# Attention with a top-32 mask, a PReLU MLP and a switch MoE on one core: ScalarE's exponentials of a pass's first group move from behind the third probability tile to behind the first

## The reference, cut to what matters

```
scores = q @ k.T / sqrt(64)                       # 4 batches x 8 heads, 576 x 576
kth    = the 32nd largest of each row
attn   = exp(scores - max) where scores >= kth, else 0
attn   = attn / (sum(attn) + 1e-9)
x      = attn @ v                                 # becomes 2304 x 512
h      = x @ w_in;  g = max(h,0) + alpha*min(h,0); x2 = g @ w_out     # 512 -> 2048 -> 512
out    = x2 (+ gate * expert_e(x2) for the rows whose skip score is positive, one of 8 experts)
```

## Time and profile before

| | |
|---|---|
| median of three runs | 1118.12 us |
| profiled execution, its own time | 1123.2 us |
| its span (first to last instruction) | 1121.4 us |
| mean granted TensorE clock | 0.934 of 2.4 GHz |
| busy: PE, DVE, ACT, POOL | 927.9, 903.8, 631.4, 427.4 us |
| shares of the span | 83%, 81%, 56%, 38% |
| idle of DVE before L1070 for the exponentials of L844 | 5.9 us in 9 waits |
| idle of PE before L560 for POOL's L1324 | 34.4 us in 19 waits |

### The profile page before, as it was taken

The page is one execution under the profiler, slowest core; times in us unless marked ns, Lnnn a source line. Parts: engine busy times, 40 slices in busy tenths (PEclk is TensorE's granted clock), DMA queues, the critical chain, the costliest instruction groups (busy, mean ns, idle before and its releaser), DMA issues.

```text
span 1121.4 us, 22533 instructions
## 1 busy us (share of the span) xinstructions
PE 927.9 (83%) x6271; PEld 616.9 (55%) x6272; DVE 903.8 (81%) x1984; ACT 631.4 (56%) x1324; POOL 427.4 (38%) x598
## 2 busy tenths in 40 slices
PE   5346588898899889888988898899888889498996
PEld 2223256675666657665766575667556567243342
DVE  4999989999999999999999999999999270611110
ACT  3786969647855785587459637954883281010100
POOL 0136738514830682267028513840582100201110
PEclk9956589999999999999999999999999799699999
DMA  7910110013002200310031004001100166626650
GB/s 205 365 37 22 32 34 22 23 41 87 0 21 70 57 0 21 96 32 21 1 97 30 21 8 119 1 21 53 44 2 1 55 226 213 221 90 225 199 165 18
DMA packets 98658, 84.05 MB, mean 75 GB/s; under 512 B 69116, under 2 KB 77308, under 8 KB 98048
## 3 DMA queue, kind: packets, MB, share of 16 engines
q1 hardware_dynamic: 94544, 78.56, 23.0%
q0 software_dynamic: 1488, 3.15, 0.8%
q10 hardware_dynamic: 2528, 1.18, 0.4%
HBM read 72.64 MB, written 11.53 MB: 75 GB/s over the span
## 4 chain that ended last, share of the span: by engine, by line
PE 62%; POOL 12%; issue 11%; ACT 8%; DVE 4%; DMA 2%; POOLq 1%; ACTq 0%; DVEq 0%
PE acc L604 16%; PE acc L571 8%; PE sc L542 7%; PE pt_full L560 6%; PE acc L590 5%; POOL pos_part L358 5%; PE sc L712 3%; PE pt_full L772 3%; POOL arena L360 3%; POOL arena L1324 2%; PE pt_full L780 2%; PE sc L721 2%; PE acc L613 2%; ACT arena L844 1%; PE acc L619 1%
## 5 line engine op out<-in xcount | busy, mean ns | idle before, releaser
L1050 DVE MAX8 best<-arena 128x8 f32<-128x576 f32 x576 | 403.5, 742 | 9.8 <-ACT arena L835 6.6
L1063 DVE MATCH_REPLACE8 arena<-best,arena 128x576 f32<-128x576 f32 x432 | 315.8, 738 | 0.0
L1324 POOL TENSOR_SCALAR arena<-arena,row_inv 128x576 f32<-128x576 f32 x144 | 106.5, 757 | 351.3 <-DVE row_inv L1082 351.3
L590 PE MATMUL acc<-arena 128*128 (+1 forms) x1536 | 202.4, 286 | 28.0 <-ACT neg_part L883 26.1
L604 PE MATMUL acc<-arena 128*128 128x288 f16 x1536 | 202.2, 289 | 2.9 <-issue 2.9
L590 PEld LDWEIGHTS acc<-arena 128*128 128x128 f16 x1536 | 146.4, 98 | 78.8 <-issue 38.9
L604 PEld LDWEIGHTS acc<-arena 128*128 128x128 f16 x1536 | 149.6, 99 | 49.6 <-issue 12.9
L560 PE MATMUL pt_full<-ident,arena 128*128 128x128 f32 x576 | 102.4, 306 | 60.0 <-POOL arena L1324 34.4
L835 ACT ACTIVATE arena<-sc 128x576 f32<-128x576 f32 x144 | 92.1, 642 | 87.1 <-PE sc L542 70.6
L1070 DVE SCALAR_TENSOR_TENSOR arena<-arena,best 128x576 f32<-128x576 f32 x144 | 126.7, 927 | 5.9 <-ACT arena L844 5.9
L560 PEld LDWEIGHTS pt_full<-ident,arena 128*128 128x128 f32 x576 | 73.1, 155 | 90.3 <-POOL arena L1324 42.9
(11 more groups left out here) (172 smaller groups left out, 942.2 us busy)
## 6 DMA issues: line engine op xcount, KB each, us to landing
arena<-in_moe_w_dram SPq DMA_DIRECT2D x64, 512.0 KB, 4.2
nat<-in_v_dram SPq DMA_DIRECT2D x64, 128.0 KB, 2.2
nat<-in_k_dram SPq DMA_DIRECT2D x60, 128.0 KB, 2.8
x_rows<-x2n SPq DMA_DIRECT2D x24, 192.0 KB, 2.4
out_dram<-x2n SPq DMA_DIRECT2D x24, 192.0 KB, 2.6
nat<-in_q_dram SPq DMA_DIRECT2D x64, 64.0 KB, 2.1
arena<-in_moe_w_in_dram SPq DMA_DIRECT2D x4, 1024.0 KB, 7.4
arena<-in_moe_w_out_dram SPq DMA_DIRECT2D x4, 1024.0 KB, 14.5
```

Of the source, the lines that this page charges most:

```text
L590: last = nc.tensor.matmul(dst[:, 0:HALF], win16[:, a, d, f * P:(f + 1) * P], xT16[:, bass.ds(row + d, 1), b, :].rearrange("p b s -> p (b s)"),
L1050: nc.vector.max(best[:, gp, j, r, :], src).then_inc(max_found if r == 0 else dve_step, 1)
L1063: nc.vector.match_replace(left[:, j, :], best[:, gp, j, r, :], src, MASKED).then_inc(dve_step, 1)
L1324: nc.gpsimd.tensor_scalar(probs[:, gp, j, :], probs[:, gp, j, :], row_inv[:, gp, j:j + 1], 1.0, ALU.mult, ALU.mult)\
```

## The change

In passes with an MLP part, ScalarE's call `exps(p, par, 0)` moves from behind the three tiles of the top to behind the first: after the store of the first probability tile and of score tile 6, ahead of the store of the second probability tile. The three exponentials, the maxima and their waits are the same. Step 0 and the other groups are not changed.

```
@@ ScalarE, step()
                             store_scores(p, par, GROUPS - 1, [j])
                             if j == 1 and not mlp:
                                 high_weights(i, par, 0, 1)
-                        if mlp:
-                            exps(p, par, 0)
+                            if j == 0 and mlp:
+                                exps(p, par, 0)
                         store_pv(p - 1, items)
```

## The result

The kernel after takes 1156.7 us (median of four runs, 1152.69 to 1161.18) against 1119.24 us before: ratio 1.0343, with an interval of 1.0309 to 1.0377. It is 37.5 us slower, where 19.6 us were forecast.

The account below looks back on a forecast made before the run. The line of TensorE, ScalarE and GpSimd handing work on, slightly longer than VectorE's, was taken to bound the kernel; 0.3 + 20.4 - 1.1 = 19.6 us on 1118.1 gave 1137.7, about 1138 us, range 1127 to 1147.

Parts of the forecast that it names:

- What bounds the kernel: Settled passes: the TensorE, ScalarE and GpSimd line is longer than VectorE's by a few tenths of a microsecond per two passes.
- Rival 4: All tops: VectorE bounds after all, delays vanish and pass 2's 3.37 us stay won, 1114.7 us; chance 0.04.
- 1.70 us per top: Each top: third tile's transposes start 3.67 us after score tile 6's store, 1.70 us late; 20.4 us over p = 3 to 14.
- None of it given back before the next top: Between tops, even to odd and odd to even: no wait absorbs the delay, so the whole 1.70 us is kept.
- p = 15 and step 7: Loop's end: TensorE's 2.13 us wait for GpSimd takes up p = 15's delay, 0 us; slack at step 7 takes off 1.1 us.
- The clock at 0: TensorE's granted clock at the tops: could not be settled, so it was entered in the sum as 0 us.
- the row at 844.40: Stretch after 2.13 us of idle time behind a PV: granted clock 0.65, four transposes take 0.98 instead of 0.66 us.
- bounds of -0.7 to +2.9 us per top: Limits given for the clock's effect at each top, with PV 5.54 us at the high clock and 8.40 in the last PV.
- rival 2: Tops: the hole also costs clock, 1.4 us per PV half; 1155 us for all tops, 1146 for half; chance 0.18.
- The hole is shorter than 2.13 us: Tops: argument against the clock falling, comparing the hole of about 1.6 us with the idle time before 844.40.
- A shift may also take away the low stretch of odd passes: Odd passes, clock 0.97: existing low-clock time may vanish when work shifts; lower bound -0.7 us per top.
- VectorE's waits: VectorE's masking: idle time grows from 5.9 to about 20 us, all at groups 1 and 2; pass 2's 3.37 us go.

Follow-up runs that it names:

- e8_occupy: Kernel before, with three added exponentials into an unused buffer at the moved call's new place, real ones staying behind the third tile: 1161.49 us, ratio 1.0372.
- e1_fill: Kernel after, with eight unused transposes of the identity on TensorE ahead of the third tile's transposes: 1149.48 us, ratio 1.0285.
- e9_fill_one: Kernel after, with one unused matmul of 512 fp32 columns in the hole ahead of the third tile's transposes: 1145.1 us, ratio 1.0226.
- e4_split: Kernel after, but only the maxima and first exponential stay behind the first tile, the other two go back behind the third: 1128.15 us, ratio 1.0075.
- e10_second: Kernel after, but with the exponentials behind the second tile and score tile 7 instead of behind the first: 1172.93 us, ratio 1.0448.
- e2_even: Kernel before with the move made in even passes only, odd passes keeping the old order: 1138.43 us, ratio 1.0169.
- e3_odd: Kernel before with the move made in odd passes only, even passes keeping the old order: 1141.07 us, ratio 1.0192.
- e11_tail: Kernel before, with three unused identity transposes behind each of the last three tiles' transposes, in the tail alone: 1123.0 us, ratio 1.0032.

## Why the prediction was wrong, point by point

- **What bounds the kernel: right.** VectorE is busy for 98 and 99% of the two passes of the earlier trace rows and is still not what sets the end. Rival 4 read those rows the other way; the passes grew by 1.6 us even where nothing else happened (54.44), and e8_occupy shows no gain from the early exponentials.
- **1.70 us per top: right.** Forecast 3.67 us from the start of the score store to the transposes, measured 3.67; forecast hole about 1.6 us, measured 1.63 to 1.64 wherever the top is reached at 2.4 GHz. The pass grew by 1.55 to 1.61 us. At p = 2, where 0.3 us were forecast, PV starts at 149.24 against 149.28: nothing lost.
- **None of it given back before the next top: right but for 0.1 us, while the clock stays.** With the clock mostly held (e1_fill), the last PV is 20.2 us late against 19.6 forecast, with the luck told there. GpSimd's third leak of the earlier trace rows shows that the line moves as a whole. Before, it started 20.45 us behind the start of PV. In p = 8 after it starts at 506.64, 21.89 us behind the PV at 484.75; the difference of 1.44 us is that PV's excess of 1.46 us.

```profile
506.64 0.80 POOL L358 TENSOR_TENSOR pos_part<-pos_part,neg_part 128x288 f32<-128x288 f32 x1 [1.05 <-ACT neg_part L886]
```

- **p = 15 and step 7: right in the balance, in part by luck.** That top has its hole of 1.63 us and a PV of 7.70 us, and still the last PV is only 35.7 us late where the PV of p = 14 was 37.1 late. The wait of 2.13 us for GpSimd is gone, the one of 1.52 us has shrunk to 0.52, and 1.4 us came back where 1.1 were forecast. But 2.2 us of slow PV were taken up as well, and the low clock that before has behind its wait (0.65 in the earlier trace rows) is 1.00 from 886 us on here; neither was in the forecast.

```profile
873.53 1.08 PE L560 MATMUL pt_full<-ident,arena 128*128 128x128 f32 x4 [1.63 <-ACT arena L857]
...
875.72 7.70 PE L571 MATMUL acc<-arena,nat 128*64 128x288 f32 x40 [0.89 <-issue]
```

- **The clock at 0: the step that failed.** The prediction had the hole, its 1.6 us, the second wait behind it, the row at 844.40 and the bounds of -0.7 to +2.9 us per top, and then put 0 into the sum. Measured: slow PVs of +1.5 to +2.5 us at seven of the twelve tops, 13.3 us in the profile, and 3.4 us as the balance of the rest; e9_fill_one takes back 14 us of the medians. 13.3 over twelve tops is 1.1 us, which happens to be the middle of those bounds; with it the sum would have given about 1151 us. It is rival 2, which stood at 0.18 with 1146 us for half of the tops and 1155 for all; the measured 1156.7 is at its upper figure, although only about half of the PVs are slow. There the sizing was short too: a slow PV was put at 1.4 us more and takes 1.5 to 2.5 more, and the routing at the low clock was not in it.
- **The reason given against rival 2 was no reason.** "The hole is shorter than 2.13 us" compared one idle stretch with one idle stretch. But the new top has two, 1.64 and 1.13 us, around 0.9 us of work. Before has single waits that are longer than the new hole and leave the clock at 1.00 in their pass, as this one in TensorE's timeline:

```profile
481.96 3.10 PE L590 MATMUL acc<-arena 128*128 x24
486.95 1.63 PE L590 MATMUL acc<-arena 128*128 x12 [1.89 <-ACT neg_part L883]
```

  So the length of a wait alone doesn't tell. Side by side, the two waits at the top were 0.30 and 1.16 us in e4_split and 0.58 and 1.13 in e9_fill_one, where the PVs from p = 3 to 15 stayed fast; 1.63 and 1.13 in the kernel after, with 12 slow of 17; and 3.17 in e10_second, all slow up to p = 14. A rule is not worked out from this: the same waits, to 0.04 us, gave six slow of six in e2_even.
- **A shift may also take away the low stretch of odd passes: right, and too small to help.** The stretch is gone in the passes from 204.04 and 541.06, whose clocks of 0.97 and 0.96 come from their slow PVs; in e4_split the clock is 1.00 in four of the six odd passes from p = 3 to 13. Each such pass wins 1.0 to 1.1 us, where the bound was -0.7, for which the prediction names no row. In other odd passes the stretch grew: the one from 315.66 has 0.87.
- **VectorE's waits.** Forecast about 20 us, all at groups 1 and 2, measured 35.5. They grow with the whole loss, the clock's part too, as those of a follower do. 4.7 us of them are at group 0 after all, in p = 6 and p = 12, whose tops are reached at the low clock.
- **Left open:** what decides from one execution to the next which PV behind a full hole is slow; and the part behind the last PV, which is between 227 and 239 us in these profiles without regard to the change.

The Trainium skill (TensorE: Matmul & The Clock Gate, "What's actually happening") gives the cost of the clock's ramp as under 1% of a typical kernel's span. That sentence is on the first matmuls of a kernel, which run at the slow clock once. No run here measures that ramp by itself; here the clock falls again at many tops, and this costs 1.25% by e9_fill_one, so the page's figure is no bound for it.

## What to carry to other kernels

When an edit makes the matmul engine wait just before a block of matmuls, the price is the wait and what the clock does to the block: read the clock by stretch around the nearest row that has such a wait, count all the idle time around that place and not the longest wait, and don't put 0 into the sum while the rows give bounds of -0.7 and +2.9. One cheap matmul without use, put into the hole, tells the two terms apart. And an early result is worth only what its taker waits for it; look first at whose store then stands behind it. One kernel shows this; that the same figures hold in another is not shown.

## What the runs showed of the hardware that was not expected

- The same hole at the same place (1.63 us, and 1.17 us behind it, p = 3) let the clock fall in one execution of the kernel after and not in another. PV behind a full hole takes 7.0 to 8.0 us in its two profiles when it falls, instead of 5.5.
- The spread of a kernel's runs says little of its clock. e3_odd's four spread over 16.3 us and e4_split's, with all PVs from p = 3 to 15 fast in its profile, over 13.0; e8_occupy's five, with nine slow PVs, over 3.1; before's twelve over 6.1, and seventeen more of it on the same chip over 11.7.
- With eight more small instructions in the loop's body, stalls of 4.5 and 4.6 us stood at the loop's turn in one profile of that kernel out of two; with one more instruction, in none (one profile).
- A faster PV near the end (2.9 us won, e11_tail) made the whole no faster: +0.32%.
